# Attention, routing and two expert networks on one core: column-tiled score and gate products, the own term's sum on TensorE, low halves of the second network moved, no filler products

## The reference, cut to what matters

```python
for t in range(S):                                  # attention: B=4, H=8, S=768, D=48
    cur = np.einsum('bhd,bhe->bhde', u[None] * kt, vt)
    y[:, :, t] = np.einsum('bhd,bhde->bhe', rt, state + cur)
    state = w[None, :, :, None] * state + np.einsum('bhd,bhe->bhde', kt, vt)
x = y.transpose(0, 2, 1, 3).reshape(3072, 384)
logits = x @ w_gate                                 # E=8 experts of 384 tokens each
# greedy assignment: best (token, expert) pair first, an expert closes at 384 tokens
h = np.maximum(x[mask] @ w1[e], 0.0); out[mask] = h @ w2[e]      # first network, 384 -> 1024 -> 384
h = np.maximum(x @ w_in, 0.0); y = (h * h) @ w_out               # second network, 384 -> 2048 -> 384
```

## Time and profile before

| | |
|---|---|
| three runs | 871.38, 870.9, 871.23 us (median 871.23) |
| the profiled execution | 872.39 us, of which the profile's span is 870.7 us |
| busy share of the span | PE 93%, PEld 89%, DVE 63%, ACT 36%, POOL 35% |
| mean granted clock of TensorE | 0.966 of full speed |
| attention | from the start to 162.5 us of the span |
| first routing and gather | 162.5 to 206.8 us |
| eight experts | 206.8 us to the end |

### The profile page before, as it was taken

How to read it: one execution, slowest core, us unless ns; L and a number is a source line. 1 busy time by engine, 2 the same in 40 slices (tenths; PEclk the granted TensorE clock), 3 DMA queues, 4 the chain that set the end, 5 groups by cost and what they waited for, 6 DMA issues and landing times.

```text
span 870.7 us, 18546 instructions
## 1 busy us (share of the span) xinstructions
PE 812.3 (93%) x6695; PEld 778.8 (89%) x6695; DVE 549.3 (63%) x1223; ACT 317.3 (36%) x693; POOL 301.0 (35%) x288
## 2 busy tenths in 40 slices
PE   5999999525999999999999999999999999999995
PEld 3999999415899999999999999999999999999995
DVE  7899999585586469456935782677458534931210
ACT  1454554212154315422542353135315432532332
POOL 6555655012035205420531153126303520541232
PEclk9999999756999999999999999999999999999998
DMA  8688876022012003100400130022001200400000
GB/s 225 205 245 245 248 235 185 20 75 98 2 73 100 28 0 105 66 27 0 168 3 27 48 123 0 27 72 99 21 6 72 99 27 1 174 1 28 2 1 27
DMA packets 22144, 69.86 MB, mean 80 GB/s; under 512 B 3552, under 2 KB 6752, under 8 KB 22112
## 3 DMA queue, kind: packets, MB, share of 16 engines
q1 hardware_dynamic: 19040, 59.99, 21.7%
q0 software_dynamic: 3072, 9.44, 3.1%
HBM read 59.98 MB, written 9.44 MB: 80 GB/s over the span
## 4 chain that ended last, share of the span: by engine, by line
PE 75%; DVE 4%; issue 1%; POOL 1%; ACT 1%; DMA 0%; DVEq 0%; ACTq 0%; POOLq 0%
PE bank L1190 16%; PE bank L1191 15%; PE bank L1192 15%; PE bank L1244 8%; PE bank L1245 8%; PE bank L1246 8%; PE bank L1137 3%; DVE hot L796 1%; PE bank L1170 1%; DVE hot L885 1%; PE bank L1159 1%; POOL xg L428 0%; DMA xg<-x_rows,perm_next 0%; POOL out L464 0%; PE bank L1143 0%
## 5 line engine op out<-in xcount | busy, mean ns | idle before, releaser
L456 POOL TENSOR_TENSOR h_lo<-sq,h_hi 128x384 fp32r<-128x384 f32 x128 | 152.9, 1197 | 398.8 <-DVE sq L960 398.7
L960 DVE SCALAR_TENSOR_TENSOR sq<-bank,relu 128x384 f32<-128x384 f32 x128 | 70.9, 554 | 133.5 <-ACT relu L554 133.2
L554 ACT ACTIVATE relu<-bank 128x384 f32<-128x384 f32 x128 | 63.1, 493 | 198.8 <-PE bank L1192 196.6
L1244 PE MATMUL bank<-m_hi,h_hi 128*128 128x384 f32 x384 | 131.9, 344 | 0.0
L1190 PE MATMUL bank<-x_hi,m_hi 128*128 128x384 f32 x384 | 130.4, 340 | 0.3
L1246 PE MATMUL bank<-m_hi,h_lo 128*128 128x384 f32 x384 | 129.6, 338 | 0.0
L1245 PE MATMUL bank<-m_lo,h_hi 128*128 128x384 f32 x384 | 129.4, 337 | 0.0
L1191 PE MATMUL bank<-x_lo,m_hi 128*128 128x384 f32 x384 | 129.1, 336 | 0.0
L1192 PE MATMUL bank<-x_hi,m_lo 128*128 128x384 f32 x384 | 129.0, 336 | 0.0
L548 ACT ACTIVATE h_hi<-bank 128x384 fp32r<-128x384 f32 x64 | 31.5, 493 | 192.4 <-PE bank L1192 192.4
L952 DVE SCALAR_TENSOR_TENSOR h_lo<-bank,h_hi 128x384 fp32r<-128x384 f32 x64 | 35.5, 554 | 71.8 <-ACT h_hi L548 71.8
(11 more groups left out here) (172 smaller groups left out, 1569.5 us busy)
## 6 DMA issues: line engine op xcount, KB each, us to landing
w_raw<-we_in SPq DMA_DIRECT2D x48, 512.0 KB, 4.4
nn<-nn_in SPq DMA_DIRECT2D x24, 576.0 KB, 4.6
tt<-tt_in SPq DMA_DIRECT2D x48, 192.0 KB, 5.1
m_raw<-m_in SPq DMA_DIRECT2D x12, 512.0 KB, 5.6
x_rows<-yrow SPq DMA_DIRECT2D x24, 192.0 KB, 2.4
xg<-x_rows,perm_next POOLq DMA_INDIRECT x24, 4.6
out<-xg,perm_now POOLq DMA_INDIRECT x24, 2.6
u_row<-u_in SPq DMA_DIRECT2D x1, 192.0 KB, 5.7
```

The costliest lines, as they stand in the source:

```text
L456: pool.tensor_tensor(h_lo[g % 3][:, :], sq[g % 2][:, :], h_hi[g % 3][:, :].bitcast(f32), ALU.subtract).then_inc(lo2_ready, 1)
L554: act.activation(relu[:, :], h_ps[g % 3][:, 0:CAP], ACT.Relu).then_inc(relu_ready, 1)
L960: dve.scalar_tensor_tensor(out=sq[g % 2][:, :], in0=h_ps[g % 3][:, 0:CAP], scalar=0.0, in1=relu[:, :], op0=ALU.max, op1=ALU.mult).then_inc ...
L1244: pe.matmul(acc_ps[t][:, 0:DM], h_hi[r][:, s], m2_hi[:, c:c + DM], start=first, stop=False)
```

## The change

- The products of `back` and `gate` are cut in two column tiles: 64 stationary columns each, with the output on PSUM partitions 0 to 63 or 64 to 127. `back` has 16 products of 64x64 in place of 8 of 128x128, `gate` 6 of 64x8 in place of 3 of 128x8.
- The own term's sum moves from DVE and POOL to PE: POOL makes r·k by head (`rk`, 112x512), and `own_term` multiplies it on PE with `u_pair`, a zero-padded u with two columns per pair of heads (8 products of 64x2). ACT copies the 8 sums out of PSUM. `rku` and `own_sum` go.
- The four fillers of `front` go.
- `nn` holds v and k only, since r by token is no longer read (576 KB become 384 KB per unit).
- The second network's raw weights get a place of their own (the one where their low halves go). Tiles 0 to 5 (w_in) are handled in the attention, one per four units: high half on ACT, low half on POOL, a quarter tile (256 columns) per unit. Tiles 6 to 11 (w_out) are loaded after the attention; their high halves are made by ACT during the routing, two low halves by POOL once the weights of expert 0 are split, and four by DVE in steps 13, 16, 18 and 21 of expert 0, whose program on DVE now stands outside the loop.

```diff
-FILL = 4
+OUT_EARLY = 2
+OUT_LOW_AT = {13: 2, 16: 3, 18: 4, 21: 5}
-        nn = [sb(f"nn{b}", [P, 3, DM], f32, att) for b in range(B)]
+        nn = [sb(f"nn{b}", [P, 2, DM], f32, att) for b in range(B)]
...
+        def out_low(eng, j):
+            eng.wait_ge(out_hi_ready, j + 1)
+            cols = slice((IN_TILES + j) * WT, (IN_TILES + j + 1) * WT)
+            return eng.tensor_tensor(m2_lo[:, cols], m2_raw[:, cols], m2_hi[:, cols].bitcast(f32), ALU.subtract)
...
             def bonus(i, b):
                 n = 4 * i + b
-                pool.tensor_tensor(rk[:, :], nn[b][:, 1, :], nn[b][:, 2, :], ALU.mult).then_inc(rk_ready, 1)
-                pool.wait_ge(rk_ready, n + 1)
-                pool.tensor_tensor(rku[j][:, :], rk[:, :], u_row[:, :], ALU.mult).then_inc(rku_ready, 1)
+                pool.wait_ge(tt_in[b], 32 * i + 32)
+                pool.wait_ge(own_made, n - 1)
+                pool.tensor_tensor(rk[b % 2][:, :, :], tt[b][:, 0, :, :], tt[b][:, 1, :, :], ALU.mult).then_inc(rk_ready, 1)
+            def in_low(i, part):
+                pool.wait_ge(in_hi_ready, i + 1)
+                cols = bass.ds(i * WT + part * (WT // B), WT // B)
+                pool.tensor_tensor(m2_lo[:, cols], m2_raw[:, cols], m2_hi[:, cols].bitcast(f32), ALU.subtract).then_inc(in_lo_ready, 1)
...
+            pool.wait_ge(w_lo_ready, WE_TILES)
+            for j in range(OUT_EARLY):
+                out_low(pool, j).then_inc(out_lo_early, 1)
...
-            def own_sum(i, b):
-            def m2_low(i, b):
...
                     rows(i, b)
-                    if not last or b < B - 1:
-                        own_sum(*one)
                     if not last:
                         state_sum(*one)
-                    m2_low(i, b)
...
+                        if is_first(i) and g in OUT_LOW_AT:
+                            out_low(dve, OUT_LOW_AT[g]).then_inc(out_lo_ready, 1)
...
-            with dve.Fori(0, E - 2) as i:
+            expert(0, False, True)
+            with dve.Fori(1, E - 2) as i:
...
-                fill(FILL, j)
...
-                        last = pe.matmul(y_ps[j][:, a, p * P:(p + 1) * P], am[j][:, a, p * P:(p + 1) * P],
-                                         nn[b][:, :, :].rearrange("p x f -> p (x f)")[:, c.start:c.start + P],
-                                         start=False, stop=p == PAIRS - 1)
+                        for t in range(0, P, HALF):
+                            last = pe.matmul(y_ps[j][t:t + HALF, a, p * P:p * P + HALF], am[j][:, a, p * P + t:p * P + t + HALF],
+                                             nn[b][:, :, :].rearrange("p x f -> p (x f)")[:, c.start:c.start + HALF],
+                                             start=False, stop=p == PAIRS - 1)
...
+            def own_term(n, j):
+                pe.wait_ge(rk_ready, n + 1)
+                for p in range(PAIRS):
+                    for t in range(0, P, HALF):
+                        last = pe.matmul(own_ps[t:t + HALF, 2 * p:2 * p + 2], rk[j][:, p, t:t + HALF], u_pair[:, p, :],
+                                         start=True, stop=True)
+                last.then_inc(own_made, 1)
...
-                    last = pe.matmul(lg_ps, yT[:, d * P:(d + 1) * P], wg[:, d, :], start=d == 0, stop=d == DC - 1)
+                    for t in range(0, P, HALF):
+                        last = pe.matmul(lg_ps[t:t + HALF, :], yT[:, d * P + t:d * P + t + HALF], wg[:, d, :],
+                                         start=d == 0, stop=d == DC - 1)
```

More of the change, by code:

```diff
@@ L133, in build @@
         kn = sb("kn", [P, DM], f32, att)
-        rk = sb("rk", [P, DM], f32, att)
-        rku = [sb(f"rku{j}", [P, DM], f32, att) for j in range(2)]
+        rk = [sb(f"rk{j}", [HD, PAIRS, P], f32, att) for j in range(2)]
         own = [sb(f"own{j}", [P, H], f32, att) for j in range(2)]
@@ L218, in build @@
         kt_ready = sem("kt_ready")
-        w_gap, tt_gap = sem("w_gap"), [sem(f"tt_gap{b}") for b in range(B)]
+        w_gap, u_gap, tt_gap = sem("w_gap"), sem("u_gap"), [sem(f"tt_gap{b}") for b in range(B)]
         w_s_in = sem("w_s_in")
@@ L305, in units @@
                         load_nn(b, 4 * i + b + 4)
-                    if not last and b % 2:
-                        sp.wait_ge(m2_lo_ready, 4 * i + b + 1)
-                        load_m2(b // 2, 2 * i + b // 2 + 2)
+                    if not last and b == 0:
+                        sp.wait_ge(in_hi_ready, i + 1)
+                        load_in(i + 1)
             with sp.Fori(0, NC - 1) as i:
@@ L498, in gated, with own_copy, own_values @@
                                ACT.Copy).then_inc(logit_ready, 1)
+            def own_copy(n, j):
+                act.wait_ge(own_made, n + 1)
+                act.activation(own[j][:, :], own_ps, ACT.Copy).then_inc(own_ready, 1)
+            def own_values(i, b):
+                n, j = 4 * i + b, b % 2
+                act.wait_ge(own_ready, n + 1)
+                act.wait_ge(nn_in[b], 16 * i + 16)
+                if not (isinstance(n, int) and n < 2):
+                    act.wait_ge(y_ready, n - 1)
+                for h in range(H):
+                    cols = slice(h * D, (h + 1) * D)
+                    done = act.activation(ownv[j][:, cols], nn[b][:, 0, cols], ACT.Copy, scale=own[j][:, h:h + 1])
+                done.then_inc(ownv_ready, 1)
             def units(i, last):
                 for b in range(B):
[L502 to L511, removed]
+                    n = 4 * i + b
+                    end = last and b == B - 1
+                    if not is_first(n):
+                        act.wait_ge(yT_sum, n)
+                    if not end:
+                        own_copy(n + 1, (b + 1) % 2)
                     if not is_first(n):
                         turned_y(n - 1)
+                    if not end:
+                        own_values(i + (b + 1) // B, (b + 1) % B)
                     if not is_first(n):
                         gated(n - 1)
-                    if b % 2 and not (last and b == B - 1):
-                        m2_high(2 * i + b // 2 + 1, 1 - b // 2, i + 1 + b // 2)
-            m2_high(0, 0, 1)
+                    if not last and b == B - 1:
+                        in_high(i + 1)
+            own_copy(0, 0)
+            own_values(0, 0)
+            in_high(0)
             units(0, False)
@@ L534, in x_high @@
                 act.activation(x_hi[:, d, :], turned(q, d), ACT.Copy).then_inc(x_hi_ready, 1)
+            for j in range(OUT_TILES):
+                act.wait_ge(out_loaded[j], 16)
+                cols = slice((IN_TILES + j) * WT, (IN_TILES + j + 1) * WT)
+                act.activation(m2_hi[:, cols], m2_raw[:, cols], ACT.Copy).then_inc(out_hi_ready, 1)
             act.wait_ge(y_ready, NU)
@@ L638, in mask @@
                                       causal[:, :].unsqueeze(1).broadcast_to([P, 4, P]), ALU.mult).then_inc(masked, 1)
-            def own_sum(i, b):
-                n, j = 4 * i + b, b % 2
-                dve.wait_ge(rku_ready, n + 1)
-                if not (isinstance(n, int) and n < 2):
-                    dve.wait_ge(ownv_ready, n - 1)
-                dve.tensor_reduce(own[j][:, :], rku[j][:, :].rearrange("p (h d) -> p h d", h=H), AX.X,
-                                  ALU.add).then_inc(own_ready, 1)
             def state_sum(i, b):
@@ L700, in _ @@
             scale(0, 1)
-            own_sum(0, 0)
             state_sum(0, 0)
@@ L1109, in units @@
                         front(i + (b + 1) // B, (b + 1) % B)
+                    if not end:
+                        own_term(n + 1, (b + 1) % 2)
                     if not is_first(n):
@@ L1238, in contract @@
                     pe.wait_ge(lo2_ready, G2 * i + g - G1 + 1)
+                    tiles = [-(-k * DM // WT) for k in (g - G1, g - G1 + 1)]
+                    if tiles[0] < tiles[1] <= OUT_EARLY:
+                        pe.wait_ge(out_lo_early, tiles[1])
+                    elif tiles[0] < tiles[1]:
+                        pe.wait_ge(out_lo_ready, tiles[1] - OUT_EARLY)
                     for t in range(TT):
```

83 lines of the change are left out of this document (46 added, 37 removed).

## The result

| | before | after |
|---|---|---|
| median of 13 runs each | 871.03 us (870.81 to 873.86) | 868.79 us (864.88 to 885.08) |
| ratio, 95% interval | | 0.9948 [0.9935, 0.9961] |
| profiled execution, span, mean clock | 872.39, 870.7 us, 0.966 | 869.18, 867.5 us, 0.946 |

The change gains about half a per cent: 2.2 us by the medians, 4.5 by the ratio, in which the run of 885 us is left out. Forecast were 854.5 us, and the time lies outside the range. The runs of the changed kernel do not agree among themselves: six are at 864.9 to 865.5, six at 868.8 to 869.4, one at 885.1. In the traces the granted clock is at 1.00 or at 0.50 (another value in a window is a mixture), so a run's mean clock says how long it was at 0.50: twice (1 - mean) times the span.

What follows compares the result with a forecast made beforehand. PE and DVE were both taken as full in the attention, PE a little more. 872.4 - 23.0 (attention) + 5.6 (expert 0) = 855.0, or 853.8 against the median; plus 0.7 for DVE's pile, 854.5 us, range 850 to 860.

Steps and rivals of the forecast that it cites:

- Attention in sum: Whole attention: 18.6 from 19 units, 1.8 from units 21 to 23, 0.9 start, 1.7 end; 23.0 us less.
- a clock of 1.00 through the attention: Attention: a listed sign that PE's granted clock stays at 1.00 in the profile after.
- DVE's pile: Expert 0, steps 13 to 18: DVE's four low halves may pile up with `w_lo`, 1 us; 0.7 added.
- should take 4.6: Attention, units 21 to 23: now 5.5 us apart, forecast at 4.6 each, saving 1.8 us.
- POOL's pieces: Attention unit on POOL: 512 columns 1.26 us, 256 columns 0.74, with the present 1.0 making 3.0 us.
- the port between DVE and POOL sets the unit: Rival, attention: POOL stops both `ks` and `rs`, unit 5.4 us, total 864; chance 0.18.
- The clock rival: Attention: clock falls without the fillers, PE's unit over 8 us at 0.5, total above 910; chance 0.03.
- Saves 0.54: PE's attention unit: dropping the fillers, from 98.41 to 98.95, saves 0.54 us.
- The tile price of 28 ns: PE's attention unit: a 64-column load costs 28 ns, so `back` takes 0.90 us for 32 loads, saving 0.89.
- the loop through PE and DVE at 4.8: Attention unit: scores, then `mask`, `ks`, `rs`, `rows` on DVE, then `front`; PE may start at 4.8 us.
- 4.3 plus 1.3 us of loss: Expert 0: 4.3 us more wait for `h_lo` behind two POOL subtractions, 1.3 for PE's low clock; 5.6 back.
- the slower rival: Attention: column tiles do not run beside each other, 56 ns a load, PE's unit 6.4 us, total 889; chance 0.06.

Runs made afterwards that it cites:

- the kernel with both repairs and fillers at the start: Changed kernel, POOL waiting for rows in the last units, two POOL subtractions before expert 0 not waiting, 22 fillers before the first two fronts: 850.97 us.
- early low halves: Changed kernel with POOL's two low halves of w_out made right behind the gather, without waiting for DVE's last `w_lo`: 863.92 us; with POOL's wait in the last units too, 852.26.
- the kernel with POOL paced: Changed kernel, POOL in the last four units waiting, before `rk` and the quarter tile, until DVE has made the rows of the unit before: 864.15 us.
- a wide `back`: Changed kernel with `back` at full width (128x128) in the first and last four units: 866.01 us; in all units, with POOL paced and early low halves: 870.65.

## Why the prediction was wrong

**The step that failed** is "Attention in sum" with the line among the things that would show it, "a clock of 1.00 through the attention". The forecast end of attention was 139.5; it came at 154.12. The runs divide the 14.7 us by the place of `best`: 9.5 for POOL's lead and the low clock behind it (150.74 against 141.20), 3.4 for the start and its low clock (154.12 against 150.74), and 1.7 for the rest, where the kernel with both repairs and fillers at the start still misses: 2.2 by 19 units of 5.01 in place of 4.9, 0.9 by the last three units and the end, less 1.3 that its warm start gains beyond the forecast. The rest of the difference in the profiles goes the other way: 5.05 came back at expert 0 where 5.6 was written, and the 0.7 for DVE's pile did not show as a loss behind expert 0's start (663.6 us with early low halves, 663.9 before).

**What was not costed.** The prediction took the last three units as plain ones ("should take 4.6"); their scores stand 6.7 and 7.8 us apart. It costed POOL's pieces only for the loop's unit, where POOL waits over 2 us for the state's products before `kn`. In the last chunk `kn` goes, and with it the wait that held POOL back. The rival "the port between DVE and POOL sets the unit" described what then happens, both operations stopped, but was asked of the middle (where `ks` is 1.07 and `rs` 0.68: it did not happen) and not of the end. The Trainium skill, page "SBUF — State Buffer", section "Who interferes with whom", says that a DVE instruction with two inputs in SBUF contends with a POOL instruction that reads SBUF, and that the lock on the port pair they share is an exclusive one. The 2.38 us of a step that needs 0.36, twice, agree.

**The clock rival.** It had a chance of 0.03, and the loss that it named is real at both ends: at the low clock a unit takes 8.66 us in the kernel with POOL paced (scores at 29.27 and 37.93) and 7.8 at the end of the changed one ("over 8"). It was put aside with one window in which PE, busy for 1.13 of 2 us, still had the high clock. Such a row shows that the clock had not fallen yet (it was down by 164), not that such work would bring it back. And the kernel before had it low at the start already, from about 24 to 27, over most of one `back`:

```profile
23.86 3.57 PE L1082 MATMUL bank<-nn,am 128*128 128x128 f32 x16
```

As it was worded, with the fillers as what holds the clock up, the rival is half right. Without them the kernel before keeps 1.00 in its loop and gains 7.7 us. With them the changed kernel has less low time in five of nine executions (61 to 68 us, against 81 and more), pays 0.36 us a unit for it, and is no faster.

**The fillers' price.** "Saves 0.54" was right for PE and for the unit almost so (5.88 to 5.43). The forecast did not ask what they alone were worth.

**What held.** The tile price of 28 ns (29 measured); `gate` 0.34 (0.35); POOL's pieces 1.26 and 0.74 (1.27 and 0.73); `ks` stopped, `rs` not; the loop through PE and DVE at 4.8 (4.84 with the loops written out, where the rows end at 65.25 and the next scores begin at 65.30); the two subtractions stopping `is_best` and `ranked`, PE's wait of 5.5 (5.00), and 4.3 plus 1.3 us of loss (5.05). The tiles run beside each other, so the slower rival is out. The Trainium skill, page "TensorEngine Tiling (Array Packing)", section "Restrictions and Gotchas", says that column tiling excludes the fast weight load; at 29 ns for a load of 64 columns against 112 for one of 128, no price of that shows here.

**What stays open.** Why the clock came back at 29.7 in one execution of the same opening code (where it fell at 19.4) and only at 56 in another (where it fell at 21.8); and whether the width of the tiles has a part in how long it stays low. The end of the attention speaks for it (7 us with a wide `back`, 22 and more with tiles), the start against it, and the experiments with a wide `back` change the width, the share of the array at work and the number of products together.

## What to carry to other kernels

A pipelined loop's last pass is a different kernel: an engine that drops a part of its work there runs ahead, and if it shares a port it can stop the engine that everything waits for, so read and cost that stretch by itself. A stall in which PE idles is worth its own length plus everything that then runs at half the clock, and how long that lasts differed here from run to run: pace the stretch so that the clock never falls. The narrow tiled products gained the most per unit, and the longest stretches at the low clock in the attention, 34 us and 22, were under them. And before a change of many parts, time the one-line part alone; here it was worth more than the whole.

## What the runs showed of the hardware

- The granted clock can stay at 0.50, which is 1.2 GHz, with PE busy nearly all the time: from 22 to about 56 us in the kernel with POOL paced (12.00 of 12.00 us busy from 40 to 52), and from 132 to the end of attention in the changed one. Apart from three transposes a unit, all these were fp32 products of 48 rows or of 48- or 64-column tiles. At the end of the attention it was back after 7 us with a wide `back` (by 143); in the changed kernel's expert 0, with full-width products, it was low at the first product at 198.5 and high by 203.8. At the start it came back after 10 us with a tiled `back` and with a full-width one alike. The Trainium skill, page "TensorE: Matmul & The Clock Gate", Part 1, has the clock follow from how busy PE is; by that and the profile's busy share the stretch from 40 to 52 should have been at 2.4 GHz, and the measurement decides.
- When POOL has several pieces ready, DVE does not always get the next turn. The `rs` of 3.13 us stands over one `rk` and, by its end at 131.16, about two quarter tiles; at expert 0 the turns alternated.
- The loops over the chunk cost 0.2 us per unit inside them (5.05 against 4.84, 16 units, 3.2 us of the time). In the profile the cost stands as 0.26 to 0.36 us of "issue" before the scores. Written out, the loops' branches, the registers' updates and the waits on a register's value went together, on all five engines, so which of them costs is not shown.
